# One split of x moved from VectorE to GpSimd and another moved past the tile's turn, in a one-core attention and two-FFN kernel

## Chip, core and metric

The kernel runs on one core of one Trainium2 chip. The metric is the device time of one execution in microseconds (us), lower is better. TensorE (PE) does the matrix products; VectorE (DVE), ScalarE (ACT) and GpSimd (POOL) do the elementwise work; SyncE (SP) issues the DMA transfers.

## What is computed

```
attn = softmax(rotate(q) @ rotate(k)^T / sqrt(64)) @ v        # 4 batches x 8 heads, 576 x 64, fp32
x    = attn as a (2304, 512) matrix
x    = (h - tanh(h)) @ w_out1,      h = x @ w_in1             # first FFN, 512 -> 2048 -> 512
out  = (h * sigmoid(h)) @ w_out2,   h = x @ w_in2             # second FFN, same sizes
```

## The kernel before

The attention part takes the first 280 us and is the same in both kernels. The rest, from there to the end, is the two FFNs. Tokens are cut into 3 tiles of 768 (`NT`, `TN`), and the 2048 hidden columns into 8 slices of 256 (`NJ`). One **group** g is one slice of one tile of one layer: 48 groups, `t = g // 8` is the tile (0 to 2 in the first layer, 3 to 5 in the second), `j = g % 8` the slice. The group with j = 0 of every tile but the first is called the tile's **turn** (groups 8, 16, 24, 32, 40); the one before it, with j = 7, is the group that works **ahead** (7, 15, 23, 31, 39).

Every fp32 operand of a product is split in a high part (a copy rounded to fp32r, made by ACT) and a low part (source minus high, made by DVE or POOL), and three products stand for one: high x low, low x high, high x high. The up product x @ w_in of a group is done with seven block products p0 to p6 instead of eight (Strassen-Winograd). So a tile of x is split once into seven parts: `x_h[i]` and `x_l[i]`, i = 0 to 6, each 128x768. Parts 0, 1 and 6 are taken from x itself (`xT`), parts 2 to 5 from sums (`xsum`), which DVE makes in `x_sum(t, k)`. Part 5's source is the last sum, `x_sum(t, 3)`, and it is written over the source of part 4, so it can be made only after `x_low(t, 4)`.

```
X_SOURCE = [("x", 0, 0), ("x", 1, 0), ("sum", 1), ("sum", 2), ("sum", 0), ("sum", 0), ("x", 1, 1)]
```

TensorE's order in group g is written out by hand (L897 to L907): p0(g), p1(g), two chunks of the down product of group g - 1, p2, one chunk, p3, one, p4, one, p5, one, p6, two. In the second layer's steady groups the down product has 12 smaller chunks, 3, 2, 1, 2, 1, 3 behind p1 to p6. In `product` (L836), p_i(g) waits for the PSUM bank: p1(g) waits for all sums of group g - 1, that is for `add_product(g - 1, 6)` on DVE, p3 for `add_product(g, 1)`, p5 for `add_product(g, 3)`. At a turn p_i waits for `x_l[i]` of its tile too (L845 to L847). The down chunks of g - 1 wait for `gate_low(g - 1, 1)` (first half) and `gate_low(g - 1, 0)` (second half).

Each engine works through its queue in the order of the program. The four queues around a turn:

- DVE (L1250 to L1286), for each group: gate(g-1,0), add 1, gate_low(g-1,0), [ahead: x_low 0 | turn: x_sum 3], add 2, [ahead: x_low 1 | turn: x_low 6], add 3, [turn: x_low 5], add 4 twice, [ahead: x_low 2, x_low 3], add 5, gate(g,1), add 6, gate_low(g,1), [ahead: x_low 4]. "add i" is `add_product(g, i)`, 128x384 from PSUM; the rest are 128x768 in SBUF.
- ACT (L1056 to L1087): copy_first(g) (p0 out of its bank), gate_high(g-1,0), [turn: x_high 6], weight_high A, D, S of group g + 1, [turn: x_high 5 behind S], weight_high O of group g, tanh(g,1), gate_high(g,1), tanh(g,0).
- POOL (L593 to L599): weight_sums of group g + 1 (four 128x256 operations, L537 to L543), then `weight_low` of A (128x512), D (128x256), S (128x1024) of group g + 1 and O (128x1024) of group g, all on L548; it has no x work after tile 0.
- SP: the loads of the weights of later groups, each waiting for the low parts that free its buffer.

The helpers record under one line each: `x_low` of DVE under L1170, `x_sum` under L1166, `x_high` under L983, `add_product` under L1218, `gate` under L1224 or L1226, `gate_low` under L1233 or L1235, POOL's `x_low` (tile 0 only) under L552. Which wait counts which low part is worked out in `x_lows` from the lists `X_POOL` and `X_DVE`.

Of the kernel before, what the change touches and what calls it, by code (L numbers as in the profile page):

```python
# [24 lines left out]
NJ = 8  # L25
# [11 lines left out]
def attention_and_two_ffn(nc, qk, vin, vfull, w_in1, w_out1, w_in2, w_out2,  # L37
                          cosq, sinq, ident, scratch, out):
    ctx = ExitStack()
    with ctx:  # L40
# [233 lines left out]
        def staged(g):  # L274

            return 32 if g < 2 else 32 + 16 * ((g - 1) // 2) if g % 2 else 64 + 16 * ((g - 2) // 2)

        def win_split(g):

            return max(w_at[x] for x in w_at if x[0] == g and x[1][0] != "O")  # L280
# [28 lines left out]
        def tile_of(g):  # L309
            return g // NJ  # L310
# [4 lines left out]
        def x_block(t, k, half):  # L315
            a = TN * (t % NT) + TH * half
            return xT[:, 2 * k:2 * k + 2, a:a + TH]
# [4 lines left out]
        def x_source(t, i):  # L322
            kind = X_SOURCE[i]
            return x_block(t, *kind[1:]) if kind[0] == "x" else xsum[kind[1]][:, :, :]


        def x_highs(t, i):
            return 7 * t + ((0, 1, 2, 3, 4, 5, 6) if t == 0 else (0, 1, 2, 3, 4, 6, 5)).index(i) + 1

        X_POOL, X_DVE = (), (0, 1, 2, 3, 4, 6, 5)  # L330

        def x_lows(t, i):

            if t == 0:
                return ("pool", i + 1) if i < 4 else ("dve", i - 3)
            if i in X_POOL:
                return "pool", 4 + len(X_POOL) * (t - 1) + X_POOL.index(i) + 1
            return "dve", 3 + len(X_DVE) * (t - 1) + X_DVE.index(i) + 1
# [159 lines left out]
        def _(pool):  # L498
# [30 lines left out]
            def weight_sums(g, part):  # L529

                t = win_s[g % 2]
                a11, a12, a21, a22 = t[:, 0:2, 0:128], t[:, 2:4, 0:128], t[:, 0:2, 128:256], t[:, 2:4, 128:256]
                if part == 0:
                    pool.wait_ge(s_wi[g % 2], staged(g))
                    if g:
                        pool.wait_ge(s_wl, win_split(g - 1))
                    nc.gpsimd.tensor_tensor(wsum[:, 0, :, :], a21, a22, ALU.add).then_inc(s_sc, 1)  # L537
                    nc.gpsimd.tensor_tensor(wsum[:, 2, :, :], a11, a21, ALU.subtract).then_inc(s_sc, 1)
                else:
                    pool.wait_ge(s_sc, 4 * g + 1)  # L540
                    nc.gpsimd.tensor_tensor(wsum[:, 1, :, :], wsum[:, 0, :, :], a11, ALU.subtract).then_inc(s_sc, 1)
                    pool.wait_ge(s_sc, 4 * g + 3)
                    nc.gpsimd.tensor_tensor(wsum[:, 3, :, :], a12, wsum[:, 1, :, :], ALU.subtract).then_inc(s_sc, 1)  # L543

            def weight_low(g, name):
                src, hi, lo = piece(g, name)
                pool.wait_ge(s_wh, w_at[g, name])
                nc.gpsimd.tensor_tensor(lo, src, hi.bitcast(F32), ALU.subtract).then_inc(s_wl, 1)  # L548
# [44 lines left out]
            for g in range(1, GROUPS):  # L593
                if g + 1 < GROUPS:
                    weight_sums(g + 1, 0)
                    weight_sums(g + 1, 1)
                    for name in ("A", "D", "S"):
                        weight_low(g + 1, name)
                weight_low(g, "O")  # L599
# [496 lines left out]
        def _(dve):  # L1096
# [52 lines left out]
            def x_sum(t, k):  # L1149

                b11, b21, b12, b22 = (x_block(t, k2, half) for half in range(2) for k2 in range(2))
                if t < NT:
                    dve.wait_ge(s_xm, (8, 12, 16)[t])
                elif t == NT:
                    dve.wait_ge(s_va, 1)
                    dve.wait_ge(s_vd, 1)
                else:
                    dve.wait_ge(s_va, t - NT + 1)
                    dve.wait_ge(s_vd, t - NT + 1)
                if k in (1, 3):  # L1160
                    dve.wait_ge(s_xt, 4 * t + k - (k == 3))
                if k == 3:
                    dve.wait_ge(s_xl, x_lows(t, 4)[1])
                o, a, b = ((xsum[0], b12, b11), (xsum[1], b22, xsum[0][:, :, :]), (xsum[2], b22, b12),
                           (xsum[0], b21, xsum[1][:, :, :]))[k]
                nc.vector.tensor_tensor(o[:, :, :], a, b, ALU.subtract).then_inc(s_xt, 1)  # L1166

            def x_low(t, i):
                dve.wait_ge(s_xh, x_highs(t, i))
                nc.vector.tensor_tensor(x_l[i][:, :, :], x_source(t, i), x_h[i][:, :, :].bitcast(F32),  # L1170
                                        ALU.subtract).then_inc(s_xl, 1)
# [39 lines left out]
            def add_product(g, i, other, to, made):  # L1211

                dve.wait_ge(s_up, 7 * g + i + 1)
                if made:
                    dve.wait_ge(s_sm, 7 * g + made)
                else:
                    dve.wait_ge(s_sn, g + 1)
                nc.vector.tensor_tensor(to, ps[:, up_bank(g, i), 0:TH], other, ALU.add).then_inc(s_sm, 1)  # L1218

            def gate(g, f):  # L1220
                h = hid[g % 2][:, f, :]
                dve.wait_ge(s_t, 2 * g + 2 - f)
                if g < NT * NJ:
                    nc.vector.tensor_tensor(h, h, th[:, f, :], ALU.subtract).then_inc(s_gf, 1)  # L1224
                else:
                    nc.vector.scalar_tensor_tensor(out=h, in0=th[:, f, :], scalar=1.0, in1=h, op0=ALU.add,  # L1226
                                                   op1=ALU.mult).then_inc(s_gf, 1)

            def gate_low(g, f):
                h = hid[g % 2][:, f, :]  # L1230
                dve.wait_ge(s_gh, 2 * g + 2 - f)
                if g < NT * NJ:
                    nc.vector.tensor_tensor(g_l[:, f, :], h, g_h[:, f, :].bitcast(F32), ALU.subtract).then_inc(s_g, 1)  # L1233
                else:
                    nc.vector.scalar_tensor_tensor(out=g_l[:, f, :], in0=h, scalar=0.5, in1=g_h[:, f, :].bitcast(F32),  # L1235
                                                   op0=ALU.mult, op1=ALU.subtract).then_inc(s_g, 1)

            def move_second(t):
                if t < NT:
                    dve.wait_ge(s_dn, 2 * NJ * (t + 1))  # L1240
                    nc.vector.tensor_copy(xT[:, 2:4, tokens(t)],
                                          flat[:, ACC + 2 * TN:ACC + 4 * TN].rearrange("p (d c) -> p d c", c=TN)).then_inc(s_vd, 1)
                else:
                    if t > NT:
                        dve.wait_ge(s_out, 16 * (t - NT))
                    dve.wait_ge(s_dn, 2 * NJ * (t + 1))
                    nc.vector.tensor_copy(ostage[:, 3:6, :], ps[:, 5:8, :]).then_inc(s_vd, 1)

            first, u2, u3, u4 = (t[:, :] for t in snap)
            for g in range(GROUPS):  # L1250
                t, j = tile_of(g), g % NJ
                ahead, turn = j == NJ - 1 and g + 1 < GROUPS, j == 0 and g
                h = hid[g % 2]
                if g:
                    gate(g - 1, 0)
                add_product(g, 1, first, h[:, 0, 0:TH], 0)
                if g:
                    gate_low(g - 1, 0)
                if NJ - 4 <= j < NJ - 1 and t + 1 < 2 * NT:
                    x_sum(t + 1, j - NJ + 4)  # L1260
                if ahead:
                    x_low(t + 1, 0)
                if turn:
                    x_sum(t, 3)
                add_product(g, 2, first, u2, 0)
                if ahead:
                    x_low(t + 1, 1)
                if turn:
                    x_low(t, 6)
                add_product(g, 3, u2, u3, 2)  # L1270
                if turn:
                    x_low(t, 5)
                add_product(g, 4, u3, h[:, 1, TH:TN], 3)
                add_product(g, 4, u2, u4, 2)
                if ahead:
                    x_low(t + 1, 2)
                if ahead:
                    x_low(t + 1, 3)
                add_product(g, 5, u3, h[:, 1, 0:TH], 3)
                gate(g, 1)  # L1280
                add_product(g, 6, u4, h[:, 0, TH:TN], 5)
                gate_low(g, 1)
                if ahead:
                    x_low(t + 1, 4)
                if j == 0 and g:
                    move_second(t - 1)  # L1286
# [62 lines left out]
```

## Time and profile before

| | |
|---|---|
| median of 3 runs | 1045.99 us (1045.75 to 1048.73) |
| the profiled execution | 1047.57 us, of it span 1045.8 us |
| busy PE / DVE / ACT / POOL | 96% / 62% / 51% / 70% |
| PE waits on record from 300 us to 1040 us | 4.2 us |
| one group | about 15.7 us |

The span is the stretch from the first to the last instruction of the trace; times in rows are counted from its start. Of an engine's row the first figure is the start, the second the duration, both in us, and the bracket at its end tells how long the engine stood idle before it and for whom. A duration includes the time in which a started instruction is held up.

### The profile page before, as it was taken

What the parts mean: (1) busy time and instruction counts of PE and PEld (TensorE: products, weight loads), DVE (VectorE), ACT (ScalarE), POOL (GpSimd) and SP (SyncE); (2) the same over time, 40 slices, a digit from 0 to 9 for tenths busy, and PEclk for the clock granted to TensorE, in tenths of its full rate; (3) what the DMA queues carried; (4) which work ended last, traced back from release to release, by engine and by line L of the source; (5) the groups of instructions that cost most, each with busy time, mean ns of one, the idle gap of its engine ahead of it and who ended that gap; (6) DMA issues with size and microseconds to landing.
All of it is one profiled execution on the core that took longest, in us unless ns stands there. A gap on an engine that the chain in (4) does not pass through costs nothing.

```text
span 1045.8 us, 17872 instructions
## 1 busy us (share of the span) xinstructions
PE 1009.0 (96%) x7116; PEld 921.0 (88%) x7116; DVE 649.1 (62%) x887; ACT 528.1 (51%) x791; POOL 731.5 (70%) x495
## 2 busy tenths in 40 slices
PE   3999999999899999999999999999999999999998
PEld 2889999999799998999989999888989889898897
DVE  6667677766555568556685466755676555764443
ACT  2667777877444354444453344543455443643432
POOL 6798999995475767756767767667668658587540
PEclk9999999999999999999999999999999999999999
DMA  5545565642212212212122122122121321223201
GB/s 178 182 124 182 153 193 158 196 141 64 56 41 81 81 42 81 64 57 81 42 81 81 41 81 80 42 81 75 47 81 42 141 81 55 67 87 107 69 21 60
DMA packets 68610, 94.56 MB, mean 90 GB/s; under 512 B 17328, under 2 KB 44208, under 8 KB 68528
## 3 DMA queue, kind: packets, MB, share of 16 engines
q1 hardware_dynamic: 68528, 93.43, 28.3%
q8 instruction: 56, 0.92, 0.4%
q14 instruction: 26, 0.21, 0.1%
HBM read 84.02 MB, written 4.79 MB: 85 GB/s over the span
## 4 chain that ended last, share of the span: by engine, by line
PE 86%; DVE 6%; POOL 3%; ACT 2%; DMA 1%; issue 1%; SPq 0%; ACTq 0%; DVEq 0%; POOLq 0%
PE ps L851 31%; PE ps L871 18%; PE ps L890 18%; PE ps L718 5%; PE ps L682 4%; PE ps L712 3%; DVE x_l L1170 2%; PE ps L620 2%; PE ps L684 1%; PE ps L672 1%; DVE hm L1102 1%; PE ps L748 1%; ACT th L1034 1%; ACT g_h L1041 1%; PE ps L638 1%
## 5 line engine op out<-in xcount | busy, mean ns | idle before, releaser
L548 POOL TENSOR_TENSOR win_l<-win_s,win_h 128x512 fp32r<-128x512 f32 x96 | 131.5, 1388 | 222.6 <-ACT win_h L974 222.6
L851 PE MATMUL ps<-x_h,win_l 128*128 128x384 f32 x672 | 227.4, 338 | 7.7 <-DVE hid L1218 4.5
L1034 ACT ACTIVATE th<-hid 128x768 f32<-128x768 f32 x96 | 80.5, 839 | 305.0 <-DVE hid L1218 305.0
L851 PE MATMUL ps<-x_l,win_h 128*128 128x384 f32 x672 | 227.6, 339 | 0.0
L851 PE MATMUL ps<-x_h,win_h 128*128 128x384 f32 x672 | 226.6, 337 | 0.0
L1218 DVE TENSOR_TENSOR hid<-ps,snap 128x384 f32<-128x384 f32 x192 | 106.3, 554 | 134.1 <-PE ps L851 133.3
L1102 DVE TENSOR_REDUCE hm<-ps 128x2 f32<-128x576 f32 x144 | 108.4, 756 | 59.4 <-PE ps L620 51.5
L851 PEld LDWEIGHTS ps<-x_h,win_l 128*128 128x128 f32 x672 | 126.6, 188 | 21.0 <-DVE hid L1218 6.4
L1218 DVE TENSOR_TENSOR snap<-ps,snap 128x384 f32<-128x384 f32 x144 | 79.5, 552 | 92.1 <-PE ps L851 92.1
L851 PEld LDWEIGHTS ps<-x_l,win_h 128*128 128x128 f32 x672 | 126.7, 189 | 10.6
L871 PE MATMUL ps<-g_h,wout_h 128*128 128x512 f32 (+1 forms) x384 | 129.9, 338 | 0.0
L871 PE MATMUL ps<-g_l,wout_h 128*128 128x512 f32 (+1 forms) x384 | 129.9, 338 | 0.0
L871 PE MATMUL ps<-g_h,wout_l 128*128 128x512 f32 (+1 forms) x384 | 129.1, 336 | 0.5 <-DVE g_l L1233 0.3
L851 PEld LDWEIGHTS ps<-x_h,win_h 128*128 128x128 f32 x672 | 126.7, 189 | 0.0
L1041 ACT ACTIVATE g_h<-hid 128x768 fp32r<-128x768 f32 x96 | 81.1, 845 | 84.9 <-DVE hid L1224 45.0
L548 POOL TENSOR_TENSOR wout_l<-wout_s,wout_h 128x1024 fp32r<-128x1024 f32 (+1 forms) x49 | 115.4, 2355 | 8.9 <-ACT wout_h L974 8.9
L548 POOL TENSOR_TENSOR win_l<-wsum,win_h 128x1024 fp32r<-128x1024 f32 (+1 forms) x50 | 119.3, 2386 | 0.0
L890 PE MATMUL ps<-wout_h,g_h 128*128 128x512 f32 x288 | 114.1, 396 | 0.0
L890 PE MATMUL ps<-wout_h,g_l 128*128 128x512 f32 x288 | 113.8, 395 | 0.0
L890 PE MATMUL ps<-wout_l,g_h 128*128 128x512 f32 x288 | 112.3, 390 | 0.7 <-DVE g_l L1235 0.5
L682 PE MATMUL ps<-hl 64*128 64x288 f32 x768 | 88.2, 329 | 0.5 <-issue 0.5
L871 PEld LDWEIGHTS ps<-g_h,wout_h 128*128 128x128 f32 x384 | 72.2, 188 | 8.1
(100 smaller groups left out, 2153.0 us busy)
## 6 DMA issues: line engine op xcount, KB each, us to landing
win_s<-w_in SPq DMA_DIRECT2D x45, 512.0 KB, 4.9
wout_s<-w_out SPq DMA_DIRECT2D x45, 512.0 KB, 3.9
raw<-qk SPq DMA_DIRECT2D x30, 576.0 KB, 4.6
v<-vfull SPq DMA_DIRECT2D x16, 384.0 KB, 4.5
R<-inverse_sums SPq DMA_DIRECT2D x32, 144.0 KB, 3.1
vr<-vin SPq DMA_DIRECT2D x16, 192.0 KB, 3.4
out<-ostage SPq DMA_DIRECT2D x2, 1536.0 KB, 8.8
ev<-ev SPq DMA_DIRECT2D x16, 144.0 KB, 5.0
```

The source lines that it names most:

```text
L548: nc.gpsimd.tensor_tensor(lo, src, hi.bitcast(F32), ALU.subtract).then_inc(s_wl, 1)
L620: last = mm(ps[:, banks + h, 0:HALF], t[a, QH, 128 * i:128 * i + 128], t[a, KH, c:c + HALF], start=True, stop=True)
L682: mm(ps[:, bank + h, 0:HALF], t[a, w, k], t[a, x, c], start=(w == KL), stop=False)
L712: last = mm(ps[:, OB + h, 0:HALF], v1[n % 2][a, WHOLE.index(i), h, :], P[whole_ring(g)][a, h, :], start=False, stop=final)
L718: last = mm(ps[:, OB + h, 0:HALF], w[n % 2][a, t, h, :], x[p][a, h, :], start=(first and m == 0), stop=False)
L851: last = mm(ps[:, up_bank(g, i), 0:TH], a[w][:, BLOCKS[i], kk, :], b[i][:, kk, :], start=(k == 0), stop=(k == 5))
L871: last = mm(flat[:, ACC + TN * d + lo:ACC + TN * d + up], x[w][:, f, 128 * d:128 * d + 128], y[:, f, lo:up], start=(j == 0 and f == 1 and ...
L890: last = mm(ps[:, 2 + c, :], y[:, f, 128 * c:128 * c + 128], x[w][:, f, :], start=(j == 0 and f == 1 and n == 0), stop=(j == NJ - 1 and f ...
L1034: nc.scalar.activation(th[:, f, :], hid[g % 2][:, f, :], ACT.Tanh, scale=(1.0, 0.5)[g // (NT * NJ)]).then_inc(s_t, 1)
L1041: nc.scalar.activation(g_h[:, f, :], hid[g % 2][:, f, :], ACT.Copy, scale=(1.0, 0.5)[g // (NT * NJ)]).then_inc(s_gh, 1)
L1102: nc.vector.tensor_reduce(o, ps[:, banks:banks + 2, 0:HALF], mybir.AxisListType.X, ALU.max, negate=True).then_inc(s_mx, 1)
L1218: nc.vector.tensor_tensor(to, ps[:, up_bank(g, i), 0:TH], other, ALU.add).then_inc(s_sm, 1)
```

## The change

In the group ahead of a turn DVE takes one low part less (`x_low(t+1, 3)` is gone). At the turn `x_low(t, 3)` stands where `x_sum(t, 3)` stood, `x_sum(t, 3)` stands where `x_low(t, 6)` stood, and `x_low(t, 6)` is given to GpSimd, behind `weight_sums` of the next group and ahead of its `weight_low`. ACT's queue, SP's and TensorE's stay as they are; the lists that the waits are counted from follow.

```
-        X_POOL, X_DVE = (), (0, 1, 2, 3, 4, 6, 5)
+        X_POOL, X_DVE = (6,), (0, 1, 2, 4, 3, 5)
...
                     weight_sums(g + 1, 0)
                     weight_sums(g + 1, 1)
+                    if g % NJ == 0:
+                        x_low(6, tile_of(g))
                     for name in ("A", "D", "S"):
                         weight_low(g + 1, name)
...
                 if turn:
-                    x_sum(t, 3)
+                    x_low(t, 3)
                 add_product(g, 2, first, u2, 0)
                 if ahead:
                     x_low(t + 1, 1)
                 if turn:
-                    x_low(t, 6)
+                    x_sum(t, 3)
                 add_product(g, 3, u2, u3, 2)
                 if turn:
                     x_low(t, 5)
...
                 if ahead:
                     x_low(t + 1, 2)
-                if ahead:
-                    x_low(t + 1, 3)
                 add_product(g, 5, u3, h[:, 1, 0:TH], 3)
```

## Rows read from the trace of the kernel before

**Rows 1.** The profile's page, part 1: busy time, share, instructions.
```profile
PE 1009.0 (96%) x7116; PEld 921.0 (88%) x7116; DVE 649.1 (62%) x887; ACT 528.1 (51%) x791; POOL 731.5 (70%) x495
```

**Rows 2.** Waits of PE, 300 to 1040 us: total us, times, longest.
```profile
PE ps L851 <- DVE hid L1218: 3.7, 5, 1.1
```

**Rows 3.** The chain that ended last: start, us, engine and line.
```profile
414.86 2.08 PE ps L851 x12
...
766.09 2.08 PE ps L890 x9
```

**Rows 4.** Timeline of PE at the turn of group 8.
```profile
397.22 0.34 PE L851 MATMUL ps<-x_h,win_l 128*128 128x384 f32 x1
...
399.50 0.44 PE L851 MATMUL ps<-x_h,win_l 128*128 128x384 f32 x1 [1.08 <-DVE hid L1218]
...
400.90 0.50 PE L871 MATMUL ps<-g_h,wout_l 128*128 128x512 f32 x1
...
405.22 0.34 PE L851 MATMUL ps<-x_h,win_l 128*128 128x384 f32 x1
...
409.43 0.34 PE L851 MATMUL ps<-x_h,win_l 128*128 128x384 f32 x1
```

**Rows 5.** Timeline of DVE, end of group 7 and the turn.
```profile
392.04 2.61 DVE L1170 TENSOR_TENSOR x_l<-xsum,x_h 128x768 fp32r<-128x768 f32 x1
...
394.57 1.49 DVE L1170 TENSOR_TENSOR x_l<-xsum,x_h 128x768 fp32r<-128x768 f32 x1
...
395.98 0.55 DVE L1218 TENSOR_TENSOR hid<-ps,snap 128x384 f32<-128x384 f32 x1
397.44 1.54 DVE L1224 TENSOR_TENSOR hid<-hid,th 128x768 f32<-128x768 f32 x1 [0.91 <-ACT th L1034]
...
403.50 0.96 DVE L1233 TENSOR_TENSOR g_l<-hid,g_h 128x768 fp32r<-128x768 f32 x1 [0.44 <-ACT g_h L1041]
404.38 0.95 DVE L1166 TENSOR_TENSOR xsum<-xT,xsum 128x768 f32<-128x768 f32 x1
...
405.71 1.59 DVE L1170 TENSOR_TENSOR x_l<-xT,x_h 128x768 fp32r<-128x768 f32 x1
```

**Rows 6.** Timeline of POOL, same stretch.
```profile
393.79 1.45 POOL L537 TENSOR_TENSOR wsum<-win_s 128x256 f32<-128x256 f32 x1
...
397.43 0.73 POOL L543 TENSOR_TENSOR wsum<-win_s,wsum 128x256 f32<-128x256 f32 x1
...
404.80 1.69 POOL L548 TENSOR_TENSOR win_l<-win_s,win_h 128x512 fp32r<-128x512 f32 x1 [6.63 <-ACT win_h L974]
...
406.45 1.45 POOL L548 TENSOR_TENSOR win_l<-win_s,win_h 128x256 fp32r<-128x256 f32 x1
407.87 3.12 POOL L548 TENSOR_TENSOR win_l<-wsum,win_h 128x1024 fp32r<-128x1024 f32 x1
```

**Rows 7.** Timeline of ACT, same stretch.
```profile
402.62 0.85 ACT L1041 ACTIVATE g_h<-hid 128x768 fp32r<-128x768 f32 x1 [1.65 <-DVE hid L1224]
403.37 0.83 ACT L983 ACTIVATE x_h<-xT 128x768 fp32r<-128x768 f32 x1
404.11 0.61 ACT L974 ACTIVATE win_h<-win_s 128x512 fp32r<-128x512 f32 x1
```

**Rows 8.** Timeline of POOL before the FFNs: a low part of x.
```profile
252.96 1.83 POOL L552 TENSOR_TENSOR x_l<-xT,x_h 128x768 fp32r<-128x768 f32 x1
```

**Rows 9.** Timelines of DVE, POOL and PE at the turns of groups 24 and 32.
```profile
652.85 0.96 DVE L1224 TENSOR_TENSOR hid<-hid,th 128x768 f32<-128x768 f32 x1 [0.91 <-ACT th L1034]
...
652.85 1.55 POOL L543 TENSOR_TENSOR wsum<-win_s,wsum 128x256 f32<-128x256 f32 x1
...
779.81 0.96 DVE L1226 SCALAR_TENSOR_TENSOR hid<-th,hid 128x768 f32<-128x768 f32 x1 [0.91 <-ACT th L1034]
...
664.26 0.34 PE L851 MATMUL ps<-x_h,win_l 128*128 128x384 f32 x1
...
791.49 0.33 PE L851 MATMUL ps<-x_h,win_l 128*128 128x384 f32 x1
```

More of the change, by code:

```diff
@@ L328, in x_highs @@
             return 7 * t + ((0, 1, 2, 3, 4, 5, 6) if t == 0 else (0, 1, 2, 3, 4, 6, 5)).index(i) + 1
-        X_POOL, X_DVE = (), (0, 1, 2, 3, 4, 6, 5)
+        X_POOL, X_DVE = (6,), (0, 1, 2, 4, 3, 5)
         def x_lows(t, i):
@@ L596, in _ @@
                     weight_sums(g + 1, 1)
+                    if g % NJ == 0:
+                        x_low(6, tile_of(g))
                     for name in ("A", "D", "S"):
@@ L1263, in _ @@
                 if turn:
-                    x_sum(t, 3)
+                    x_low(t, 3)
                 add_product(g, 2, first, u2, 0)
@@ L1268, in _ @@
                 if turn:
-                    x_low(t, 6)
+                    x_sum(t, 3)
                 add_product(g, 3, u2, u3, 2)
@@ L1276, in _ @@
                     x_low(t + 1, 2)
-                if ahead:
-                    x_low(t + 1, 3)
                 add_product(g, 5, u3, h[:, 1, 0:TH], 3)
```

## Prediction

> **What bounds the kernel.** I read the page first: PE is busy 96% of the span [rows 1]. Then PE's waits over the FFNs: five of the six recorded are for DVE's sums at L1218, 3.7 us together, none longer than 1.1 [rows 2]. There is one at each turn. The chain that ended last is PE alone in the other groups and leaves it only there, for DVE. A product takes 1.04 us and a first-layer down chunk 1.05, a second-layer one 0.70 (half of 2.08; a third of 2.08) [rows 3]. So the edit can give back only the turns' losses, and can lose time only where it makes PE wait.
>
> The turn of group 8 shows the loss. p0(8) starts at 397.22 and p1(8) could follow at 398.26; it starts at 399.50, 0.06 behind the end of add 6 of group 7, and the chunk behind it at 400.90 instead of 400.54 [rows 4]. Add 6 is late because DVE holds two `x_low` from 392.04 to 396.06, and add 5, tanh, gate(7,1) and add 6 are queued behind them [rows 5]. With restarting PE, 0.12 (a first spacing of 0.28 for 0.17), the turn loses about 1.7 us.
>
> **How DVE and GpSimd hold each other up.** This prices everything below. An operation of 128x768 takes DVE 0.95 us free. The `x_low` begun at 392.04 took 2.61, the next one 1.49 [rows 5]; GpSimd's 128x256 operation begun at 393.79 took 1.45, one begun at 397.43 took 0.73 [rows 6]. The ends line up: `x_low` at 394.65, GpSimd's at 395.24, the next `x_low` at 396.06. They run one after another, whole, and the one held up ends its free time less 0.13 after the other: 0.59, 0.82. The order is that of asking: at 394.57 DVE issued its second `x_low`, but GpSimd had been waiting since 393.79 and went first. The other way round, the `x_low` issued at 405.71 [rows 5] went ahead of GpSimd's D, issued at 406.45 behind its own A [rows 6]: ends 406.49, 407.30, 407.90. Adds, with one input in PSUM, are not held up (0.55) [rows 5].
>
> The Trainium skill's "SBUF — State Buffer", section "Who interferes with whom", has the same lock for a VectorE instruction with two SBUF inputs, and its section "A bandwidth-pool intuition that's wrong" puts GpSimd's start about 0.115 us behind VectorE's end, where the rows put it 0.13 ahead. By the page each of the three handovers from DVE to GpSimd below would come some 0.25 later, and the sum over five turns would be about 3.7 us larger. I go by the rows.
>
> **Part 1: one `x_low` less in group 7.** The first `x_low` still ends at 394.65. Add 5 starts at 394.57 instead of 395.98, 1.41 earlier, and gate(7,1) at 396.03, as far behind add 5 as before (1.46) [rows 5]. There GpSimd is in its third sum: its four of 0.73 less overlap end at 395.24, 395.95, 396.65, so the gate ends at 397.46 against 398.98. Everything that hangs from it on DVE and ACT comes 1.52 earlier. Add 6 then ends by 397.95, before p1's slot; gate_low(7,1) ends at 399.33 against p1's end at 399.30, and the chunk starts at 399.42. The old loss is gone but for 0.1. At turns 24 to 40 GpSimd's last sum did not get in front of the gate [rows 9], so there the gate ended earlier already, and the shift is only 0.94 to 0.95.
>
> **Part 2: `x_low(8, 3)` at the turn.** It was 4.5 us ahead of its reader and now is due for p3(8), whose slot is 399.42 + 4.20 = 403.62 (405.22 less 400.90, less a restart) [rows 4]. DVE reaches it where it reached `x_sum`, 404.38 less 1.52 = 402.86 [rows 5]. Free it would end at 403.81, 0.2 late.
>
> **Part 3: `x_low(8, 6)` on GpSimd.** Its price is 1.83 us free [rows 8], against DVE's 0.95. It waits for `x_high` of part 6, which ACT ended at 404.20 [rows 7]; GpSimd starts 0.08 behind ACT (404.72 to 404.80) [rows 6, 7], so at 404.28, or 402.76 in the new time. That is 0.10 **before** DVE issues `x_low(8, 3)`, and inside gate_low(7,0), which ends at 404.46, or 402.94 [rows 5]. Both hang from the same gate_high, so this order is the same at all turns. By the rule above GpSimd goes first and the low part that PE needs goes second:
>
> - GpSimd's part 6 ends at 402.94 + 1.70 = 404.64; `x_low` 3 at + 0.82 = 405.46.
> - p3(8) starts at 405.52, 1.9 late.
>
> **Part 4: the sum, then part 5, two places later.** `x_sum(8, 3)` now stands behind add 2. A of `weight_low` was waiting and goes first: 405.46 + 1.16 = 406.62. The sum ends + 0.82 = 407.44, D + 0.60 = 408.04. ACT's `x_high` 5 needs 0.83 and two steps of 0.03, so DVE issues `x_low` 5 at 408.35. GpSimd has issued S, which takes 2.40 free (2.27 behind `x_low` 5 in the old order, 408.72 to 410.99) [rows 6], at 408.01, 0.34 before. S ends at 410.41, `x_low` 5 at 411.23, and p5(8) starts at 411.29 where it started at 409.43 [rows 4]. With PE's restart that is **+1.98** for the turn, the old loss already counted off. In the new order p5's slot behind the late p3 is 405.52 + 0.12 + 4.21 = 409.85, so the second stall is 1.4.
>
> What hides the rest: GpSimd then ends S at 410.41 and O near 412.8, no later than before (410.99 for S), since its queue started 1.5 earlier; so the weight loads that SP issues upon them are not later, and p0(9), 5.2 behind p5, near 416.6, has its weights. Part 6 is there 7 us before p6. x's high parts and the buffers of parts 3, 5 and 6 are not needed again in that tile. ACT's O waits behind `x_high` 5 until 408.3; it needs to be there for 410.4.
>
> **The sum.** From the end of gate(g-1,1) to the end of `x_low` 5 there are 411.23 less 397.46 = 13.77 us. Turns 8 and 16: +1.98 each. Turn 24: gate issued at 652.85 less 1.41, ends 1.43 later at 652.87; p5 at 652.87 + 13.77 + 0.18 = 666.82 against 664.26 [rows 9]: +2.56. Turns 32 and 40: gate ends at 779.83, p5 at 793.78 against 791.49 [rows 9]: +2.29 each. Together 3.96 + 2.56 + 4.58 = **+11.1 us**. The profiled execution took 1047.57; against the median of 1045.99 this gives **1057.1 us**, 1.1% slower.
>
> **Rivals.**
> - *Only the first stall.* If `x_low` 5 gets in before S (it has to be issued 0.34 us sooner relative to it), the loss is that at p3: 405.52 + 0.12 less 405.22 = 0.42 at turns 8 and 16. p3 starts 8.06 + 0.12 behind the gate's end: turn 24 661.05 against 664.26 less 4.21, +1.0; turns 32 and 40, where p3 to p5 is 1.04 + 0.70 + 1.04 + 1.39 = 4.17, 788.01 against 787.32, +0.7. Sum +3.2: 1049.2 us. For it: only 0.34 decides. Against: all steps hang from one chain.
> - *DVE goes first at the turn* (the other side). The place is `x_low` 3 against GpSimd's part 6; it decides once GpSimd asks 0.10 us later than I put it, or if DVE, following itself, keeps its turn. Then `x_low` 3 ends at 403.81, part 6 at 405.51, the sum at 406.33, A at 407.49, `x_low` 5 at 408.31: 10.85 behind the gate. p5 comes at 408.49 against 409.43, -0.94 twice; 663.90, -0.36; 790.86, -0.63 twice. Sum -3.5: 1042.5 us. For it: the two lie close, as at 397.43 and 397.44, where GpSimd went first, and at 652.85 for both, where DVE did [rows 5, 6, 9]. Against: 0.10 is ten times that difference, and GpSimd waits inside DVE's earlier operation, as at 393.79.
> - *No wait of its own: the whole gain.* 3.7 of waits, and 0.65 at each turn for the late chunk and restart (1.73 less 1.08): -7.0, 1039.0 us. It takes GpSimd holding nobody up, against the rows.
> - *One more hold.* If one more GpSimd operation of 0.7 (as the 128x256 ones) gets in front of DVE at each turn, 5 x 0.7 = 3.5 us come on top: 1060.6 us. No row shows a place for it.
>
> **How the numbers follow.** Chances: both stalls 0.64, one stall 0.13, DVE first 0.13, whole gain 0.05, one more hold 0.05. The predicted time is the first case's. The range leaves out DVE first and the whole gain (0.18) and holds one stall with 3 us below it for a shorter first stall, and one more hold at the top: 1046 to 1061. 0.3% (3.1 us) is about what a measurement can tell from no change: faster (under 1042.9) has DVE first for the most part and the whole gain, 0.16; the same has some of one stall, at its edge, and of DVE first, 0.12; slower 0.72.
>
> **What the new profile would show.** PE's wait for L1218 at the turn gone; at each turn two waits of PE's products for L1170, near 1.9 and 1.4 (less in the second layer for the first). GpSimd's new L552 row near 1.9, started 0.1 before DVE's `x_low` row of some 2.6, and S at 2.4 with a DVE `x_low` row of near 2.9 beside it. I am wrong if the DVE row is near 0.95 and GpSimd's near 2.6 (DVE went first), or if part 5's is short.

## The result and the profile after

The changed kernel takes 1056.87 us (median of 3, 1056.79 to 1057.15) against 1045.99: ratio 1.0105, interval 1.0085 to 1.0125. On another chip, beside later runs, it was 1057.13 against 1046.17: 1.0104, interval 1.0091 to 1.0118. So it is 1% slower, some 11 us; 1057.1 was forecast.

In the changed kernel the lines from L597 on to VectorE's loop stand two further down, in the kernels of the runs by up to five. The page's row of busy time answers to [rows 1], the list of PE's waits over the FFNs to [rows 2]:

```profile
PE 1007.9 (96%) x7116; PEld 919.7 (87%) x7116; DVE 658.1 (62%) x882; ACT 528.9 (50%) x791; POOL 737.0 (70%) x500
```

```profile
PE ps L853 <- DVE x_l L1172: 14.5, 10, 1.8
```

PE's work is the same. Its five waits for the sums at L1218 (3.7 us) are gone, and ten waits for low parts of x (14.5 us) have come: two at each of the five turns. The timeline of the turn of group 8, PE first, then DVE, then GpSimd, answers to [rows 4 to 6] and [rows 8]:

```profile
403.53 0.41 PE L853 MATMUL ps<-x_h,win_l 128*128 128x384 f32 x1 [1.75 <-DVE x_l L1172]
409.25 0.41 PE L853 MATMUL ps<-x_h,win_l 128*128 128x384 f32 x1 [1.29 <-DVE x_l L1172]
...
392.50 0.55 DVE L1220 TENSOR_TENSOR hid<-ps,snap 128x384 f32<-128x384 f32 x1
393.96 1.43 DVE L1226 TENSOR_TENSOR hid<-hid,th 128x768 f32<-128x768 f32 x1 [0.92 <-ACT th L1036]
...
399.92 0.96 DVE L1235 TENSOR_TENSOR g_l<-hid,g_h 128x768 fp32r<-128x768 f32 x1 [0.45 <-ACT g_h L1043]
400.79 2.59 DVE L1172 TENSOR_TENSOR x_l<-xsum,x_h 128x768 fp32r<-128x768 f32 x1
...
403.77 1.57 DVE L1168 TENSOR_TENSOR xsum<-xT,xsum 128x768 f32<-128x768 f32 x1
...
406.34 2.77 DVE L1172 TENSOR_TENSOR x_l<-xsum,x_h 128x768 fp32r<-128x768 f32 x1 [0.53 <-ACT x_h L985]
...
400.70 1.88 POOL L552 TENSOR_TENSOR x_l<-xT,x_h 128x768 fp32r<-128x768 f32 x1 [4.71 <-ACT x_h L985]
...
405.90 2.39 POOL L548 TENSOR_TENSOR win_l<-wsum,win_h 128x1024 fp32r<-128x1024 f32 x1
```

Read the two x_l rows of DVE beside GpSimd's. GpSimd issued part 6 at 400.70, 0.09 before DVE issued part 3 at 400.79 (0.09 to 0.10 at all five turns); GpSimd's took 1.88, DVE's 2.59 instead of 0.95, and p3 started at 403.53, 0.15 behind its end. GpSimd issued S at 405.90, DVE part 5 at 406.34; S took 2.39, part 5 2.77, and p5 started at 409.25. PE's two waits are 1.75 and 1.29; 1.9 and 1.4 were forecast.

These times stand in another frame than those of before: the FFNs began 2.06 us earlier in this execution. The chain shows it at the first down chunk, here and then in the kernel before:

```profile
286.90 2.36 PE ps L873 x12
```

```profile
288.96 2.37 PE ps L871 x12
```

So p5(8) at 409.25 is 411.31 in the frame of before; 411.29 was forecast. The spans differ by 1054.7 - 1045.8 = 8.9 us only, because of these 2.06; from the first down chunk to the end it is 767.8 against 756.8, +11.0. That stretch is called the FFN stretch below, and is in the table for every kernel, since the start of the FFNs moves by up to 3.7 us from one profiled execution to the next whatever the kernel.

### The profile page after: what moved, and what is told of

Same layout as the page of the kernel before. It is cut to its first block, busy times and chain, and to the rows that moved or that the text cites. A ratio compares the mean times of both kernels' runs of the same rounds, so it can differ in the third digit from the quotient of the medians.

```text
span 1054.7 us, 17872 instructions
## 1 busy us (share of the span) xinstructions
PE 1007.9 (96%) x7116; PEld 919.7 (87%) x7116; DVE 658.1 (62%) x882; ACT 528.9 (50%) x791; POOL 737.0 (70%) x500
## 4 chain that ended last, share of the span: by engine, by line
PE 82%; DVE 8%; POOL 3%; ACT 3%; issue 3%; DMA 1%; SPq 0%; ACTq 0%; DVEq 0%; POOLq 0%
PE ps L853 29%; PE ps L892 17%; PE ps L873 16%; PE ps L720 5%; PE ps L684 4%; PE ps L714 4%; DVE x_l L1172 3%; PE ps L622 2%; PE ps L686 1%; PE ps L674 1%; PE ps L750 1%; DVE hm L1104 1%; ACT g_h L1043 1%; DVE hid L1226 1%; DVE xsum L1168 1%
## 5 line engine op out<-in xcount | busy, mean ns | idle before, releaser
L548 POOL TENSOR_TENSOR win_l<-win_s,win_h 128x512 fp32r<-128x512 f32 x96 | 132.7, 1401 | 202.0 <-ACT win_h L976 202.0
L853 PE MATMUL ps<-x_h,win_l 128*128 128x384 f32 x672 | 226.9, 338 | 17.8 <-DVE x_l L1172 14.5
L548 POOL TENSOR_TENSOR wout_l<-wout_s,wout_h 128x1024 fp32r<-128x1024 f32 (+1 forms) x49 | 119.3, 2435 | 8.9 <-ACT wout_h L976 8.9
L548 POOL TENSOR_TENSOR win_l<-wsum,win_h 128x1024 fp32r<-128x1024 f32 (+1 forms) x50 | 115.7, 2314 | 0.0
```

What stands on the lines that cost most here:

```text
L853: last = mm(ps[:, up_bank(g, i), 0:TH], a[w][:, BLOCKS[i], kk, :], b[i][:, kk, :], start=(k == 0), stop=(k == 5))
```

## The experiments

Three readings were set against each other. **Order of asking**: DVE and GpSimd run operations with two inputs in SBUF one after another, whichever asks first; the edit makes DVE ask second at both places that PE waits for. **Place alone**: part 3 at the turn is late by itself. **GpSimd's load**: its queue is 1.8 us longer at a turn, and something behind it is late.

"O" is GpSimd's `weight_low` of O. In the table "before beside it" is the kernel before, timed beside that run. The chips differ by up to 1.2 us for that kernel, so runs are compared by what each loses or gains against it; the last columns are of the one profiled execution of each kernel.

| kernel | median us | before beside it | ratio (95%) | span - first chunk = FFN stretch | against before's 756.8 |
|---|---|---|---|---|---|
| changed, again | 1057.13 | 1046.17 | 1.0104 (1.0091 to 1.0118) | 1054.4 - 286.6 = 767.8 | +11.0 |
| 1 GpSimd's part alone | 1051.74 | 1046.94 | 1.0043 (1.0031 to 1.0055) | 1047.6 - 287.8 = 759.8 | +3.0 |
| 2 part 6 asks later | 1049.25 | 1046.94 | 1.0024 (1.0015 to 1.0034) | 1047.8 - 288.7 = 759.1 | +2.3 |
| 3 S behind part 5 | 1051.89 | 1046.94 | 1.0049 (1.0037 to 1.0060) | 1049.0 - 286.8 = 762.2 | +5.4 |
| 4 part 6 behind S | 1050.91 | 1046.94 | 1.0040 (1.0028 to 1.0052) | 1047.8 - 287.9 = 759.9 | +3.1 |
| 5 part 6 later, O held | 1043.72 | 1045.74 | 0.9983 (0.9975 to 0.9992) | 1043.5 - 289.8 = 753.7 | -3.1 |
| 6 part 3 in the tanh gap | 1042.96 | 1045.74 | 0.9983 (0.9974 to 0.9991) | 1040.5 - 287.5 = 753.0 | -3.8 |
| 7 tanh gap, O held | 1043.00 | 1045.74 | 0.9974 (0.9963 to 0.9984) | 1040.9 - 287.8 = 753.1 | -3.7 |
| 8 GpSimd takes part 3 | 1045.96 | 1045.74 | 1.0003 (0.9995 to 1.0012) | 1044.1 - 288.7 = 755.4 | -1.4 |
| 9 gap, sum held | 1040.37 | 1046.17 | 0.9949 (0.9936 to 0.9963) | 1037.2 - 286.1 = 751.1 | -5.7 |

Every kernel has the same 3978 matmul instructions from the first down chunk on, so their starts can be set against those of the kernel before, one by one, both counted from that chunk. But for less than 0.1 us in all, the difference changes only at the turns. Summed over the five turns, in us, it grows by:

| kernel | up to p2 (the old wait at p1) | p2 to p4 (p3's wait) | p4 to the end of p6 (p5's wait) | from there to behind the first down chunk of the turn's own group |
|---|---|---|---|---|
| the change | -5.9 | +9.2 | +7.6 | 0.0 |
| 1 GpSimd's part alone | -1.2 | +1.1 | +0.5 | +2.5 |
| 2 part 6 asks later | -5.9 | +1.0 | +1.5 | +5.8 |
| 3 S behind part 5 | -5.9 | +9.2 | +0.1 | +1.9 |
| 4 part 6 behind S | -5.9 | +1.0 | +7.7 | +0.2 |
| 5 part 6 later, O held | -5.9 | +1.0 | +1.4 | +0.3 |
| 6 part 3 in the tanh gap | -3.9 | 0.0 | 0.0 | 0.0 |
| 7 tanh gap, O held | -4.0 | 0.0 | 0.0 | +0.3 |
| 8 GpSimd takes part 3 | -6.0 | 0.0 | +2.3 | +2.3 |
| 9 gap, sum held | -5.7 | 0.0 | 0.0 | 0.0 |

**1. GpSimd's part alone.** The kernel before, with

```
-        X_POOL, X_DVE = (), (0, 1, 2, 3, 4, 6, 5)
+        X_POOL, X_DVE = (6,), (0, 1, 2, 3, 4, 5)
...
+                    if g % NJ == 0:
+                        x_low(6, tile_of(g))        # POOL, behind weight_sums
...
                 if turn:
-                    x_low(t, 6)                     # DVE, behind add 2
```

> The kernel before, with only part 6 given to GpSimd; part 3 keeps its place in the group ahead. Order of asking: p1 waits as before (1.1 at turn 8); GpSimd's part 6 gets in front of x_sum 3 (1.7 later), which no product needs at once; add 2 behind it comes 0.2 too late for p4, part 5 is in time. +0.3 us a turn, 1047.6 us. Place alone (part 3 at the turn is the whole cost): 1046 us. GpSimd's load (1.8 us more in its queue makes weights late): near 1057 us, with PE waiting for L548.

Measured 4.8 us slower, 3.2 more than expected. Timeline of it at the turn of group 8:

```profile
402.62 2.61 DVE L1168 TENSOR_TENSOR xsum<-xT,xsum 128x768 f32<-128x768 f32 x1
...
410.69 2.68 DVE L1226 TENSOR_TENSOR hid<-hid,th 128x768 f32<-128x768 f32 x1 [0.91 <-ACT th L1036]
...
402.53 1.89 POOL L552 TENSOR_TENSOR x_l<-xT,x_h 128x768 fp32r<-128x768 f32 x1 [4.71 <-ACT x_h L985]
...
410.14 2.41 POOL L548 TENSOR_TENSOR wout_l<-wout_s,wout_h 128x1024 fp32r<-128x1024 f32 x1
...
415.73 0.47 PE L873 MATMUL ps<-g_h,wout_l 128*128 128x512 f32 x1 [0.27 <-ACT xT L1050]
```

The sum met part 6 as expected (2.61 for 0.95), and the 0.3 a turn expected of it is there (+1.1 and +0.5 in the second table). What I had not followed is the next meeting: O, issued at 410.14, held gate(8,1), issued at 410.69, for 1.7. O was ahead of that gate in the kernel before too, but further ahead, and held it for 1.1:

```profile
412.17 2.01 DVE L1224 TENSOR_TENSOR hid<-hid,th 128x768 f32<-128x768 f32 x1 [0.92 <-ACT th L1034]
...
410.96 2.40 POOL L548 TENSOR_TENSOR wout_l<-wout_s,wout_h 128x1024 fp32r<-128x1024 f32 x1
```

ACT's high part of the gate and its move of the tile's outputs come behind it, and the first down chunk waits for the move. In runs 1 and 2 that chunk starts 2.36 behind the gate's end. By the same 2.36 it could have started at 416.54 in the kernel before, where it started at 416.78 without a wait: an estimate of 0.24 us of slack. Run 1 used it up, and loses 2.5 us there over the five turns.

Part of what run 1 loses is hidden behind a near tie. At turns 8 and 16 gate(g-1,1) and GpSimd's fourth weight sum are issued within 0.01 us of each other, here (both at 396.27 at turn 8) as in the kernel before. There the sum went first (397.43 and 397.44 [rows 5, 6]); here the gate did and took 0.96, so that PE waited 0.50 at p1 instead of 1.08. That is the -1.2 in the second table, and no run tells whether the tie falls the same way in every execution.

Run 1 thus loses 4.8 us by the medians and 3.0 in the FFN stretch, of 11: giving part 6 away costs something in itself, but the larger part needs both halves of the edit. No PE wait names L548, so the weights are not late.

**2. Part 6 asks later.** The changed kernel, with

```
                     if g % NJ == 0:
+                        pool.wait_ge(s_wh, w_at[g + 1, "A"])
                         x_low(6, tile_of(g))
```

> The changed kernel, with one more wait: GpSimd's part 6 waits for ACT's high part A of the next weights too, 0.6 us later, so that VectorE's part 3 asks for its inputs first. The work is the same. Order of asking: part 3 takes 0.95 instead of 2.6, S no longer beats part 5 by a whole operation, both waits of PE at the turn shrink from 1.8 and 1.3 to about 0.2 each: 1042.5 us (the rival 'DVE goes first', worked out before). Place alone: part 3 still sits at the turn, 1055 us or more. GpSimd's load: the same or a little slower than 1057 us.

```profile
402.54 0.95 DVE L1173 TENSOR_TENSOR x_l<-xsum,x_h 128x768 fp32r<-128x768 f32 x1
...
407.00 0.98 DVE L1173 TENSOR_TENSOR x_l<-xsum,x_h 128x768 fp32r<-128x768 f32 x1 [0.53 <-ACT x_h L986]
...
410.92 3.18 DVE L1227 TENSOR_TENSOR hid<-hid,th 128x768 f32<-128x768 f32 x1 [0.92 <-ACT th L1037]
...
402.97 2.22 POOL L552 TENSOR_TENSOR x_l<-xT,x_h 128x768 fp32r<-128x768 f32 x1 [5.23 <-ACT win_h L977]
...
410.89 2.40 POOL L548 TENSOR_TENSOR wout_l<-wout_s,wout_h 128x1024 fp32r<-128x1024 f32 x1
...
416.46 0.47 PE L874 MATMUL ps<-g_h,wout_l 128*128 128x512 f32 x1 [0.53 <-ACT xT L1051]
```

This timeline is the sharpest test: the same work with one wait more, and the kernel loses 2.3 us against the one before instead of 10.9 by the medians; its FFN stretch is 8.7 us shorter than the changed kernel's. GpSimd's part 6 is issued 0.43 behind part 3 instead of 0.09 ahead of it. Part 3 now asks first and takes 0.95 where it took 2.59; part 5 takes 0.98 where it took 2.77. "Place alone" and "GpSimd's load" both fail here: what part 3's place at the turn costs by itself is at most the +1.0 up to p4 in the second table. The total of 1042.5 fails too: 3.5 less than before was expected, 2.3 more was measured. O was issued at 410.89, the gate at 410.92. Going second, the gate took 2.2 us longer, and the down chunk waits for ACT's move behind it: +5.8 in the last column of the second table.

**3. S behind part 5.** The changed kernel, with

```
                     for name in ("A", "D", "S"):
+                        if name == "S" and g % NJ == 0:
+                            pool.wait_ge(s_xl, x_lows(tile_of(g), 5)[1])
                         weight_low(g + 1, name)
```

> The changed kernel, with one more wait: at a turn GpSimd's S waits until VectorE has made part 5. Order of asking: the wait of 1.8 us at p3 stays, the one of 1.3 at p5 goes: +3.2 us on before, 1049.2 us (the rival 'only the first stall'). Place alone: no change from 1057 us. GpSimd's load: slower than 1057 us, since its queue is held up more.

```profile
PE ps L855 <- DVE x_l L1174: 8.1, 5, 1.8
```

PE's list of waits shows the second wait of each turn gone and the first still there, in size as before: 8.1 us in five waits where there were 14.5 in ten. The kernel loses 5.0 us against the one before instead of 10.9. That is 1.8 us more than expected. O, issued 0.83 ahead of the gate, holds it longer here as well (2.40 in its timeline, 2.01 before), and the second table has 1.9 us for it.

**4. Part 6 behind S.** The changed kernel, with part 6 of GpSimd moved behind the three low parts of the weights:

```
-                    if g % NJ == 0:
-                        x_low(6, tile_of(g))
                     for name in ("A", "D", "S"):
                         weight_low(g + 1, name)
+                    if g % NJ == 0:
+                        x_low(6, tile_of(g))
```

> The changed kernel, with GpSimd's part 6 moved behind A, D and S of the next weights. Order of asking: part 3 takes 0.95 and p3 waits 0.2 at most, but A gets in front of the sum and S in front of part 5, which ends 12.1 us behind the gate instead of 13.8: p5 waits some 1.4. +0.3 at turns 8 and 16, +0.9 at 24, +0.6 at 32 and 40: 1048.8 us. Place alone: 1055 us or more. GpSimd's load: 1057 us or less by little, since the weights come first.

```profile
401.82 0.95 DVE L1172 TENSOR_TENSOR x_l<-xsum,x_h 128x768 fp32r<-128x768 f32 x1
...
405.73 2.77 DVE L1172 TENSOR_TENSOR x_l<-xsum,x_h 128x768 fp32r<-128x768 f32 x1 [0.53 <-ACT x_h L985]
...
405.29 2.39 POOL L548 TENSOR_TENSOR win_l<-wsum,win_h 128x1024 fp32r<-128x1024 f32 x1
...
408.65 0.41 PE L853 MATMUL ps<-x_h,win_l 128*128 128x384 f32 x1 [1.29 <-DVE x_l L1172]
```

The mirror image of run 3: part 3 is free, p3 doesn't wait, and S (405.29) still goes ahead of part 5 (405.73), which takes 2.77; p5 waits 1.29. The FFN stretch is +3.1, the medians differ by 4.0; +2.8 was expected. Runs 3 and 4 take away one of the two waits each.

**5. Part 6 later, O held.** Run 2, with

```
+                if g % NJ == 0:
+                    pool.wait_ge(s_gf, 2 * g + 1)
                 weight_low(g, "O")
```

> The kernel in which part 6 asks later, with one more wait of GpSimd's: at a turn O stands back until VectorE has made gate(g,1). There that gate took 3.18 us instead of 0.95, behind an O issued 0.03 us before it, and TensorE then waited 0.5 for ACT's move of the tile's outputs. Order of asking: the gate takes 0.95, that wait is gone, and the time is what was worked out for the rival 'DVE goes first', 3.5 us less than before: 1043.4 us. If GpSimd's load were the reason: slower than 1049 us, since its queue is held up more. If part 3's place at the turn costs by itself: 1049 us.

```profile
412.07 0.96 DVE L1229 TENSOR_TENSOR hid<-hid,th 128x768 f32<-128x768 f32 x1 [0.91 <-ACT th L1039]
...
413.11 2.42 POOL L548 TENSOR_TENSOR wout_l<-wout_s,wout_h 128x1024 fp32r<-128x1024 f32 x1 [1.02 <-DVE hid L1229]
```

The gate takes 0.96 instead of 3.18 and PE waits at no turn. 3.5 us less than before was worked out for "DVE goes first"; the FFN stretch is 3.1 shorter, the medians differ by 2.0 (1043.72 to 1045.74). The part of run 2's time that had not been expected was O ahead of the gate: the last column falls from 5.8 to 0.3. This kernel has every operation of the changed one, on the same engines and in the same queues, and against the kernel before beside each it is 13 us better; it differs by two waits of GpSimd's.

**6. Part 3 in the tanh gap.** A version that takes the gain without its price: the kernel before, with

```
-                if ahead:
-                    x_low(t + 1, 3)
                 add_product(g, 5, u3, h[:, 1, 0:TH], 3)
+                if ahead:
+                    x_low(t + 1, 3)
                 gate(g, 1)
```

> The kernel before with one edit: in the group ahead, part 3's low part moves behind add 5, into the 0.91 us in which VectorE stands idle for the tanh. Order of asking: add 5 starts 1.4 earlier as in the changed kernel, part 3 runs in the gap and the gate still ends with it, since GpSimd's sum held it up anyway; the turn itself is untouched. The wait at p1 goes, and nothing new comes but up to 0.4 at gate_low where GpSimd's last sum gets in front: -1.3 to -1.7 at turns 8 and 16, -0.7 to -1.1 at the other three: 1040.5 us. If the place in the group ahead were what costs: 1046.9 us as before.

```profile
393.17 0.55 DVE L1218 TENSOR_TENSOR hid<-ps,snap 128x384 f32<-128x384 f32 x1
393.64 1.02 DVE L1170 TENSOR_TENSOR x_l<-xsum,x_h 128x768 fp32r<-128x768 f32 x1
394.63 1.44 DVE L1224 TENSOR_TENSOR hid<-hid,th 128x768 f32<-128x768 f32 x1
...
396.99 1.32 DVE L1233 TENSOR_TENSOR g_l<-hid,g_h 128x768 fp32r<-128x768 f32 x1 [0.45 <-ACT g_h L1041]
...
396.75 0.74 POOL L543 TENSOR_TENSOR wsum<-win_s,wsum 128x256 f32<-128x256 f32 x1
...
398.37 0.50 PE L871 MATMUL ps<-g_h,wout_l 128*128 128x512 f32 x1 [0.30 <-DVE g_l L1233]
```

The gate took 1.44, as in the changed kernel (1.43), and DVE did part 3 in the gap on top. p1 no longer waits. 2.8 us faster than before by the medians (1.8 by the ratio), 3.8 in the FFN stretch; 5.5 were expected. One wait is left at each turn, for which the expectation had allowed 0 to 0.4: GpSimd's fourth sum was issued at 396.75, 0.24 before gate_low, and PE waits 0.30.

**7. Tanh gap, O held.** Run 6 with the wait of run 5.

> The kernel with part 3 in the tanh gap, and O at a turn held until VectorE has made gate(g,1), as in the other run. O then no longer gets in front of that gate, but there TensorE has slack of more than 1 us: the same time as with part 3 in the tanh gap alone, within 1 us; 1040.5 us.

1043.00 us, FFN stretch 753.1 against 753.0: no difference. In run 6 O still went ahead of gate(8,1), which took 1.98; here it took 0.96, and the time is the same. O ahead of the gate costs nothing where PE's next reader has the slack; it is not a cost by itself.

**8. GpSimd takes part 3.** The kernel before, with

```
-        X_POOL, X_DVE = (), (0, 1, 2, 3, 4, 6, 5)
+        X_POOL, X_DVE = (3,), (0, 1, 2, 4, 6, 5)
...
+                if g % NJ == 0:
+                    x_low(3, tile_of(g))            # POOL, ahead of weight_sums
...
-                if ahead:
-                    x_low(t + 1, 3)                 # DVE
```

> The kernel before, with part 3 instead of part 6 given to GpSimd, in front of weight_sums of the next group, in the stretch in which GpSimd later stands idle for 6.6 us. Order of asking: it is ready 7 us before p3 and meets the gate for 0.3 only; the weight sums run 1.8 later into gate_low, part 4 and gate(g-1,0), so that the chain of the turn starts 0.5 earlier than before instead of 1.5: p5 -1.0 at turns 8 and 16, -0.4 at 24, -0.7 at 32 and 40: 3.8 us less than before, 1043.1 us. If GpSimd's load were the cost of the change: near 1057 us.

```profile
393.48 2.58 POOL L552 TENSOR_TENSOR x_l<-xsum,x_h 128x768 fp32r<-128x768 f32 x1
...
410.86 2.49 DVE L1226 TENSOR_TENSOR hid<-hid,th 128x768 f32<-128x768 f32 x1 [0.91 <-ACT th L1036]
...
410.14 2.40 POOL L548 TENSOR_TENSOR wout_l<-wout_s,wout_h 128x1024 fp32r<-128x1024 f32 x1
```

The same extra load on GpSimd, in another place, costs nothing on balance (ratio 1.0003). It gained 1.4 in the FFN stretch instead of 3.8. Up to the end of p6 it gained 3.7, near what was expected (-6.0 at p1, +2.3 at p5); the other 2.3 went at the first down chunk, for O (410.14) was again only a little ahead of the gate (410.86).

**9. Gap and sum held.** Run 6, with the fourth weight sum of a turn held back:

```
                     pool.wait_ge(s_sc, 4 * g + 3)
+                    if g > 1 and g % NJ == 1:
+                        pool.wait_ge(s_gf, 2 * (g - 1))
                     nc.gpsimd.tensor_tensor(wsum[:, 3, :, :], a12, wsum[:, 1, :, :], ALU.subtract).then_inc(s_sc, 1)
```

> The kernel with part 3 in the tanh gap, with one more wait of GpSimd's: around a turn its fourth weight sum (L543) stands back until VectorE has made gate(g-1,0), and so no longer asks 0.24 us before gate_low(g-1,1). It then runs while VectorE has only an add and a wait for ACT. Order of asking: gate_low takes 0.96 instead of 1.32, the wait of 0.3 at the first down chunk of each turn goes, with its restart 0.4 x 5 = 2 us less than with the tanh gap alone: 1041 us. If TensorE's 0.3 had another cause: no change from 1043 us.

```profile
395.51 0.96 DVE L1235 TENSOR_TENSOR g_l<-hid,g_h 128x768 fp32r<-128x768 f32 x1 [0.45 <-ACT g_h L1043]
...
398.35 0.74 POOL L545 TENSOR_TENSOR wsum<-win_s,wsum 128x256 f32<-128x256 f32 x1 [3.15 <-DVE hid L1226]
```

gate_low takes 0.96, GpSimd's sum 0.74 in the stretch where DVE waits for ACT, and no wait of PE's is on record at any turn: 1040.37 us, 0.5% faster than before and 1.6% faster than the changed kernel. It is the fastest of the study.

**The changed kernel again**, beside run 9.

> The changed kernel as it is, on the chip of the run beside it, for the size of the change in more rounds: 10.5 us more than before, 1056.5 us.

11.0 us more than before, 1057.13.

## Why the prediction was right, point by point

- **Order of asking.** Right, and shown: moving GpSimd's request by 0.5 us against DVE's (run 2) turned part 3's 2.59 into 0.95. The margin was put at 0.10, and is 0.09 (400.70 to 400.79). The sign of the result hung on that tenth: with GpSimd second and O out of the way (run 5) the kernel is faster than before.
- **Part 1** (gate at 393.96 took 1.43, add 5 to gate 1.46): as worked out. p1 no longer waits.
- **Parts 2 and 3.** p3(8) was put at 405.52; it is 403.53 + 2.06 = 405.59.
- **Part 4.** p5(8) was put at 411.29; it is 411.31. S was to be issued 0.34 ahead of part 5, and was 0.44 ahead (405.90 to 406.34). Runs 3 and 4 show that the two waits are separate, one from part 6, one from S.
- **The other turns.** The timeline of PE has p5 of groups 24 and 32 at:

```profile
668.57 0.41 PE L853 MATMUL ps<-x_h,win_l 128*128 128x384 f32 x1 [1.30 <-DVE x_l L1172]
...
798.09 0.41 PE L853 MATMUL ps<-x_h,win_l 128*128 128x384 f32 x1 [1.28 <-DVE x_l L1172]
```

  In the frame of before (2.06 later), and against p5's starts in [rows 9], the losses piled up to there are 6.37 and 8.66; forecast were 3.96 + 2.56 = 6.52 and 6.52 + 2.29 = 8.81, in which PE's restart of 0.12 behind p5 is already counted. The FFN stretch grew by 11.0, forecast 11.1.
- **What I had wrong without harm.** O was put to end near 412.8; it ended at 411.37 + 2.06 = 413.4, since it was issued behind a waiting part 5 and took 3.12. It has slack there.
- **The handover.** The Trainium skill's "SBUF — State Buffer", section "A bandwidth-pool intuition that's wrong", gives its 115 ns for a DMA transfer whose descriptors GpSimd writes. Carried over to GpSimd's own operations, as the prediction tried it (each handover to GpSimd 0.25 later, 3.7 us more in all), it gives an estimate of 1060.8. The measured total and p5's start (411.31, 411.29 by the rows) agree with the rows, not with that estimate.
- **The rival "DVE goes first" was priced wrong.** Its condition was right, but its 1042.5 left out O ahead of gate(8,1): the chain comes earlier, O does not, and the gate is held for 2.2 us where it was held for 1.1. Under that condition the kernel takes 1049.25 (run 2); its gain needs O held as well (run 5, 3.1 us in the FFN stretch). Its sum stopped at p5, and the next meeting lies behind it; up to there it was right (-5.9 + 1.0 + 1.5 = -3.4 in the second table, -3.5 forecast). Runs 1 and 8 were misjudged for the same reason.
- **"Only the first stall"** was put at 1049.2 and measured 1051.89 in run 3. Against the kernel before, +3.2 was forecast and +5.4 found in the FFN stretch. Up to the end of p6 the second table has +3.4; the other 1.9 us come at the first down chunk, behind the same gate held by O (2.40).
- **The whole gain of 7.0** was read rightly, and run 9 reached 5.7 of it. In an ordinary first-layer group PE needs 2.08 us from p0's start to the chunk behind p1, and 2.10 for that chunk; over the five turns of the kernel before these stretches are 6.9 us longer together, by PE's timeline. Run 9 still has 1.1 of them. At each turn the chunk starts 0.1 late or little more, too short for a row in the list of waits, and then takes PE's restart, at turn 8 0.12 (0.34 between its first two matmuls, at 396.53 and 396.87, for 0.23).

What stays open: whether the near ties of run 1 fall the same way in every execution, which would move the kernels that have them by up to 1.2 us. Each kernel has one trace here, the changed one two.

## What to carry to other kernels

When work moves between VectorE and GpSimd, or along VectorE's queue, list for both engines the moments at which each operation with two SBUF inputs is issued: the later one pays the whole of the earlier one, so that tenths of a microsecond in the order of issue decide over 1 to 2 us. Follow such a sum past the first consumer that it reaches, to the end of the next group: a hold that used to lie in slack grows when VectorE's chain comes earlier and the other engine's operation does not. In these runs the cure was cheap: put the operation where VectorE idles for another engine anyway (run 6), or hold GpSimd's back by a semaphore wait on something that VectorE or ACT does just before (runs 2, 5 and 9).

## What the runs showed of the hardware

The hold goes by order of issue, in both directions. In the FFNs of the twelve traces some 2350 pairs of a VectorE 128x768 operation with two SBUF inputs and a GpSimd operation overlap; wherever one was issued more than 0.05 us ahead of the other, it went first. An engine already waiting goes ahead of an operation that the other issues back to back behind its own (the second `x_low` at 394.57, with GpSimd waiting since 393.79 [rows 5, 6]). At all five turns of run 2, O led the gate by 0.02 to 0.04 us and went first, which cost VectorE 2.2 us each time. Below 0.05 us the recorded order is no sure guide: in the changed kernel VectorE's gate was issued at 687.44 and GpSimd's next sum, back to back behind its own, at 687.48, and the gate took 1.60, behind it; leads under 0.015 us fell either way. The longest single cost seen is run 2's 3.18 us for a gate that takes 0.96 free. Adds with one input in PSUM took 0.54 to 0.56 next to any of this. The Trainium skill's "SBUF — State Buffer", section "Who interferes with whom", says "Issue order, not op shape, decides who blocks"; run 2 and the changed kernel agree, 0.95 and 2.59 for the same operation.
